# Two MLP channel mixers behind attention: the up projections as seven block products instead of eight, on chunks of 768 tokens

## The chip, the cores and the metric

One core of one Trainium2 chip. The metric is device time of the whole launch in microseconds (us); lower is better. Three runs of the kernel before lie between 791.92 and 793.27 us.

## The reference

Clustered attention on q, k, v of shape (2, 8, 768, 64), then two mixers on the result x (2 batches x 768 tokens x 512 channels), all in fp32:

```python
def _moe_ref(x, U, V, w_ch1, w_ch2):          # w_ch1 512 x 2048
    xt = x.transpose(0, 2, 1)
    u = x + (xt @ U @ V).transpose(0, 2, 1)   # rank 32
    return u + np.maximum(u @ w_ch1, 0.0) @ w_ch2
def _moe2_ref(x, w_tok1, w_tok2, w_ch1, w_ch2):   # w_ch1 512 x 1536
    xt = x.transpose(0, 2, 1)
    h = np.maximum(xt @ w_tok1, 0.0) @ w_tok2     # 768 -> 256 -> 768
    u = x + h.transpose(0, 2, 1)
    return u + np.maximum(u @ w_ch1, 0.0) @ w_ch2
```

The change concerns the products `u @ w_ch1` (the "up" matmuls), and with them everything in the function `mixers`. Attention is the same in both kernels.

## The kernel before

A product of fp32 numbers is made from three passes: each operand is split into a high part (rounded to the matmul's fp32r type, by ScalarE, `ACT`) and a low part (the rest, by VectorE, `DVE`), and TensorE (`PE`) adds high x high, high x low and low x high into one PSUM bank of 512 columns.

The mixers follow each other. Each begins with token mixing (L957, L976: L940 transposes the resulting u into `uT`), and goes on to its channel mixer in three chunks of 512 tokens (`CHUNK`). In a chunk a loop runs over the blocks f of 128 hidden units, 16 of them in the first mixer and 12 in the second. `up(f)` (L989) makes 12 matmuls of 512 columns into one of two banks `hid`; ACT writes relu of it as `h_hi` (L1067), DVE `h_lo` (L1126); `down(f)` (L998) makes 12 matmuls of 512 columns into four accumulators `acc`. The loop is written with the ups one block ahead: up(f+1), down(f), up(f+2), down(f+1). So 84 blocks pass, with 1008 up and 1008 down matmuls. Weights of each block come by two DMAs of 256 KB from SyncE's queue (`SP`, L882 and L884) into double buffers, and are split by ACT (L1039, L1069) and DVE (L1089, L1130). The hidden layer lives for one block only. At the end of a chunk DVE adds the four accumulators to x (L1150). GpSimd (`POOL`) splits V and the token weights (L906 to L919) at the start and tiles of x for the second mixer (L926, L928), far ahead of their use. All order is by hand: each engine has its own list, with semaphores between them.

## Time and profile before

| | |
|---|---|
| median of 3 runs | 792.05 us |
| the profiled execution | 792.6 us |
| its span, first to last instruction | 790.7 us |
| PE busy in the span | 97% |
| DVE, ACT, POOL busy | 57%, 46%, 17% |
| mixers: first PE matmul to the last DVE add | from 269.1 to 788.2 us |

1.9 us of the profiled execution lie around its span. In the profile a matmul's busy time is longer than its turn, since matmuls overlap in the array: what counts is the distance between the starts of one and the next.

### The profile page before, as it was taken

Reading aid. Unit: us, or ns where it says so; the run is one execution under the profiler, and the core shown is the slowest. Engines: PE = TensorE matmul, PEld = TensorE weight load, DVE = VectorE, ACT = ScalarE, POOL = GpSimd, SP = SyncE. Lnnn points to the kernel's source line nnn. Section 1 sums busy time; section 2 is a strip of 40 time slices with the busy share of each in tenths; the row PEclk is TensorE's granted clock in tenths of the full one; section 3 lists DMA queues with packets and bytes.
Section 4 is the critical chain, followed back from the end, with each engine's and each line's share of the span. In section 5 each row is a group of like instructions: output and inputs, shape, how many; then the busy total and the mean of one; then the engine's idle time right before and its main releaser. Section 6 shows DMA issues by size and latency. Waiting matters only on the chain.

```text
span 790.7 us, 12902 instructions
## 1 busy us (share of the span) xinstructions
PE 768.8 (97%) x3997; PEld 659.8 (83%) x3997; DVE 450.1 (57%) x761; ACT 361.7 (46%) x742; POOL 136.0 (17%) x162
## 2 busy tenths in 40 slices
PE   7989999999999889999999999999999999999998
PEld 6878999999999668888888888888888888888886
DVE  4778999999999684333533353334254335334333
ACT  5567888888888533323333233332123233323321
POOL 1351332233228660000300040000300000000000
PEclk9999999999999999999999999999999999999999
DMA  7935354444441223333323323333003333333334
GB/s 246 225 105 134 94 122 103 119 105 119 105 117 33 70 96 101 93 105 83 104 80 106 99 84 110 88 98 106 0 1 107 93 93 94 93 106 84 103 105 173
DMA packets 82840, 81.08 MB, mean 103 GB/s; under 512 B 7296, under 2 KB 69056, under 8 KB 82816
## 3 DMA queue, kind: packets, MB, share of 16 engines
q1 hardware_dynamic: 82816, 80.77, 37.0%
q8 instruction: 14, 0.23, 0.1%
q14 instruction: 10, 0.08, 0.0%
HBM read 56.95 MB, written 4.72 MB: 78 GB/s over the span
## 4 chain that ended last, share of the span: by engine, by line
PE 63%; DVE 2%; ACT 0%; issue 0%
PE bank L998 29%; PE bank L989 29%; PE bank L976 2%; PE bank L957 2%; PE bank L940 1%; DVE kT_hi L1099 1%; DVE x L1117 0%; DVE x L1150 0%; DVE w_lo L1130 0%; DVE uT_lo L1094 0%; DVE w_lo L1089 0%; DVE t L1108 0%; DVE h_lo L1126 0%; ACT qT_hi L1048 0%; ACT h_hi L1067 0%
## 5 line engine op out<-in xcount | busy, mean ns | idle before, releaser
L1126 DVE SCALAR_TENSOR_TENSOR h_lo<-bank,h_hi 128x512 fp32r<-128x512 f32 x84 | 58.1, 692 | 261.8 <-ACT h_hi L1067 261.8
L1067 ACT ACTIVATE h_hi<-bank 128x512 fp32r<-128x512 f32 x84 | 50.2, 598 | 301.4 <-PE bank L989 301.4
L989 PE MATMUL bank<-uT_hi,w_hi 128*128 128x512 f32 x336 | 131.2, 391 | 0.0
L998 PE MATMUL bank<-w_hi,h_hi 128*128 128x512 f32 x336 | 131.1, 390 | 0.0
L989 PE MATMUL bank<-uT_hi,w_lo 128*128 128x512 f32 x336 | 130.8, 389 | 0.0
L989 PE MATMUL bank<-uT_lo,w_hi 128*128 128x512 f32 x336 | 130.8, 389 | 0.0
L998 PE MATMUL bank<-w_hi,h_lo 128*128 128x512 f32 x336 | 130.7, 389 | 0.0
L998 PE MATMUL bank<-w_lo,h_hi 128*128 128x512 f32 x336 | 130.7, 389 | 0.0
L595 DVE TENSOR_TENSOR pT_lo<-back,pT_hi 128x384 fp32r<-128x384 f32 x192 | 98.1, 552 | 6.9 <-ACT pT_hi L496 3.5
L496 ACT ACTIVATE pT_hi<-back 128x384 fp32r<-128x384 f32 x192 | 84.4, 497 | 36.2 <-PE back L740 34.6
L563 DVE TENSOR_REDUCE negmax<-front 128x1 f32<-128x768 f32 x96 | 91.3, 952 | 9.2 <-PE front L639 9.2
L447 ACT ACTIVATE prob<-front,negmax 128x768 f32<-128x768 f32 x96 | 87.9, 916 | 1.2 <-DVE negmax L563 1.2
L740 PE MATMUL back<-ident,prob 128*128 128x128 f32 x576 | 79.3, 274 | 0.4 <-DVE pT_lo L595 0.4
L989 PEld LDWEIGHTS bank<-uT_hi,w_hi 128*128 128x128 f32 x336 | 63.1, 188 | 13.5 <-DVE uT_lo L1094 0.4
L998 PEld LDWEIGHTS bank<-w_hi,h_hi 128*128 128x128 f32 x336 | 63.1, 188 | 13.2 <-issue 0.2
L998 PEld LDWEIGHTS bank<-w_hi,h_lo 128*128 128x128 f32 x336 | 63.1, 188 | 13.1
L989 PEld LDWEIGHTS bank<-uT_hi,w_lo 128*128 128x128 f32 x336 | 63.0, 188 | 13.1
L989 PEld LDWEIGHTS bank<-uT_lo,w_hi 128*128 128x128 f32 x336 | 63.1, 188 | 12.9
L998 PEld LDWEIGHTS bank<-w_lo,h_hi 128*128 128x128 f32 x336 | 63.1, 188 | 12.9
L740 PEld LDWEIGHTS back<-ident,prob 128*128 128x128 f32 x576 | 68.4, 141 | 2.7 <-DVE pT_lo L595 0.6
L758 PE MATMUL back<-pT_hi,v_split 128*128 128x384 f32 x192 | 67.9, 354 | 0.8 <-DVE pT_lo L595 0.6
L760 PE MATMUL back<-pT_lo,v_split 128*128 128x384 f32 x192 | 64.8, 337 | 0.0
(125 smaller groups left out, 1054.1 us busy)
## 6 DMA issues: line engine op xcount, KB each, us to landing
w_raw<-in_moe_w_ch_dram SPq DMA_DIRECT2D x168, 256.0 KB, 2.9
Q<-qT_hi SPq DMA_DIRECT2D x64, 96.0 KB, 2.2
K<-kT_hi SPq DMA_DIRECT2D x64, 96.0 KB, 2.1
q_raw<-in_q_dram SPq DMA_DIRECT2D x8, 384.0 KB, 6.0
k_raw<-in_k_dram SPq DMA_DIRECT2D x8, 384.0 KB, 7.0
Q<-qT_lo SPq DMA_DIRECT2D x32, 96.0 KB, 2.1
K<-kT_lo SPq DMA_DIRECT2D x32, 96.0 KB, 2.1
v_raw<-in_v_dram SPq DMA_DIRECT2D x16, 192.0 KB, 2.7
```

Source lines behind the costliest of these rows:

```text
L447: nc.scalar.activation(prob[t % 2][:, :], s_slot[t % 2], ACT.Exp, bias=negmax[:, t % TPP:t % TPP + 1], accum_out=sums[:, t % TPP:t % TPP + ...
L496: nc.scalar.activation(pT_hi[G % 2][:, HT * half:HT * half + HT, P * (t % GT):P * (t % GT) + P], t_bank[n % 3][:, 0:HT * P].rearrange("p ( ...
L563: nc.vector.tensor_reduce(negmax[:, t % TPP:t % TPP + 1], s_slot[t % 2], AX.X, ALU.max, negate=True).then_inc(max_done, 1)
L595: nc.vector.tensor_tensor(pT_lo[G % 2][own], t_bank[n % 3][:, 0:HT * P].rearrange("p (n c) -> p n c", c=P), pT_hi[G % 2][own].bitcast(F32) ...
L740: last = nc.tensor.transpose(t_bank[i % 3][:, t * P:(t + 1) * P], prob[n % 2][:, c:c + P], ident[:, :])
L758: nc.tensor.matmul(av_bank, v_sp[j][:, token_of(t), :], pT_hi[n % 2][:, t, :], start=(t == 0), stop=False)
L760: last = nc.tensor.matmul(av_bank, v_sp[j][:, token_of(t), :], pT_lo[n % 2][:, t, :], start=False, stop=(t == NT - 1))
L957: last = nc.tensor.matmul(bank_of(L, n)[:, :], w, y[:, i, :], start=(t == 0 and m == 0), stop=(t == NT - 1 and m == len(pairs) - 1))
L989: last = nc.tensor.matmul(hid[par][:, :], w[par][:, kd, :], y[cc % 2][:, kd, :], start=(kd == 0 and m == 0), stop=(kd == KD - 1 and m == 2))
L998: last = nc.tensor.matmul(acc[k][:, :], y[par][:, k * P:(k + 1) * P], w[par][:, :], start=(start and m == 0), stop=(stop and m == 2))
L1067: nc.scalar.activation(h_hi[par][:, :], hid[par][:, :], ACT.Relu).then_inc(h_hi_made, 1)
L1126: nc.vector.scalar_tensor_tensor(out=h_lo[par][:, :], in0=hid[par][:, :], scalar=0.0, in1=h_hi[par][:, :].bitcast(F32), op0=ALU.max, op1=A ...
```

## The change

The chunks become the two batches of each mixer, four chunks `cc` of 768 tokens, and each is done in two phases. In the first, all up products of the chunk: two blocks of 128 hidden units (a pair, `p`; 8 pairs in each chunk of the first mixer, 6 in the second) form, with the two halves of the 512 channels and of the 768 tokens, a product of 2x2 by 2x2 blocks, done by Strassen's scheme in Winograd's form: seven products q of 6 matmuls of 384 columns (42 a pair) with sums on either side. POOL makes the four sums of weight blocks in place (`pair_sums`, L975 to L980), ACT and DVE split all seven in one and two instructions (`a_high`, `a_low`); four sums of blocks of uT and the split of seven (`moving_...`) are made once a chunk, by DVE and ACT for the first, by POOL alone for the three others. A product goes to one of six banks in turn; ACT copies the first (`snap`) and DVE adds the others into `h`, by 7 additions of 384 columns (`combine`). `h` keeps the chunk's whole hidden layer. In the second phase (`down`) each block is split (`hs_hi`, `hs_lo`, 768 columns) and 18 matmuls of 512 columns follow, into six banks. Token mixing and transposes of the next chunk are put between the products of this one (`pieces`: TF the first token matmuls, TS the second, TR the transposes; two banks, 6 and 7, are theirs); for that, POOL splits tiles of x (`stage`) and the second token weights (`second_weights`, two times now). The core of the diff, with indents shortened:

```diff
-            def down(f, par, start=False, stop=False):
-                wait(pe, w2_made, n0 + f + 1)
-                wait(pe, h_made, n0 + f + 1)
-                for k in range(TPC):
-                    for m, (y, w) in enumerate(((h_hi, w2_hi), (h_hi, w2_lo), (h_lo, w2_hi))):
-                        last = nc.tensor.matmul(acc[k][:, :], y[par][:, k * P:(k + 1) * P], w[par][:, :],
-                                                start=(start and m == 0), stop=(stop and m == 2))
-                    if stop:
-                        last.then_inc(acc_mm, 1)
...
-            with pe.Fori(0, nf[L] // 2 - 1) as i:
-                up(i * 2 + 2, 0)
-                down(i * 2 + 1, 1)
-                up(i * 2 + 3, 1)
-                down(i * 2 + 2, 0)
...
-            def rest(f, par):
-                dve.wait_ge(h_hi_made, n0 + f + 1)
-                nc.vector.scalar_tensor_tensor(out=h_lo[par][:, :], in0=hid[par][:, :], scalar=0.0,
-                                               in1=h_hi[par][:, :].bitcast(F32),
-                                               op0=ALU.max, op1=ALU.subtract).then_inc(h_made, 1)
-                dve.wait_ge(w2_hi_made, n0 + f + 1)
-                nc.vector.tensor_tensor(w2_lo[par][:, :], w2_raw[par][:, :],
-                                        w2_hi[par][:, :].bitcast(F32), ALU.subtract).then_inc(w2_made, 1)
...
+def pieces(cc):
+    at = {}
+    if cc == 0:
+        for t in range(NT):
+            at[3 + 2 * t] = [("TR", NT + t)]
+    elif cc < 3:
+        first = 6
+        for t in range(NT):
+            at[first + t] = [("TF", t)]
+            at[first + NT + 2 + t] = ([("TR", NT * (cc + 1) + t - 1)] if t > 0 else []) + [("TS", NT * (cc + 1) + t)]
+        at[first + 2 * NT + 2] = [("TR", NT * (cc + 1) + NT - 1)]
+    return at
...
+    def load_pair(cc, p):
+        n = pbase[cc] + p
+        w3 = layers[cc // B][0].rearrange("(k p) f -> p k f", p=P)
+        wait(sp, a_made, 2 * (n - 1))
+        for i in range(2):
+            f0 = (2 * p + i) * P
+            sp.dma_start(a_raw[n % 2][:, 2 * i:2 * i + 2, :, :].rearrange("p s k c -> p (s k) c"),
+                         w3[:, :, f0:f0 + P]).then_inc(w1_in[n % 2], 16)
...
+        load_w2(cc, 0, 0)
+        load_w2(cc, 1, 1)
+        if cc + 1 < NCH:
+            load_pair(cc + 1, 0)
+            load_pair(cc + 1, 1)
+        with sp.Fori(1, nf[cc] // 2) as i:
+            load_w2(cc, i * 2, 0)
+            load_w2(cc, i * 2 + 1, 1)
...
+    def pair_sums(cc, p):
+        n = pbase[cc] + p
+        raw = a_raw[n % 2]
+        pool.wait_ge(w1_in[n % 2], (n // 2 + 1) * 32)
+        nc.gpsimd.tensor_tensor(raw[:, 4, :, :], raw[:, 2, :, :], raw[:, 3, :, :], ALU.add).then_inc(sums_made, 1)
+        pool.wait_ge(sums_made, 4 * n + 1)
+        nc.gpsimd.tensor_tensor(raw[:, 5, :, :], raw[:, 4, :, :], raw[:, 0, :, :], ALU.subtract).then_inc(sums_made, 1)
+        nc.gpsimd.tensor_tensor(raw[:, 2, :, :], raw[:, 0, :, :], raw[:, 2, :, :], ALU.subtract).then_inc(sums_made, 1)
+        pool.wait_ge(sums_made, 4 * n + 2)
+        nc.gpsimd.tensor_tensor(raw[:, 6, :, :], raw[:, 1, :, :], raw[:, 5, :, :], ALU.subtract).then_inc(sums_made, 1)
...
+    def moving_split(cc, q):
+        if q in BC_SUM:
+            pool.wait_ge(bc_sum, 4 * cc + BC_SUM[q])
+        nc.gpsimd.tensor_copy(bc_hi[:, q, :, :], bc_block[q]).then_inc(bc_hi_made, 1)
+        pool.wait_ge(bc_hi_made, PRODS * cc + q + 1)
+        nc.gpsimd.tensor_tensor(bc_lo[:, q, :, :], bc_block[q], bc_hi[:, q, :, :].bitcast(F32),
+                                ALU.subtract).then_inc(bc_made, 1)
...
+    def moving_blocks(cc):
+        pool.wait_ge(uT_made, NT * (cc + 1))
+        pool.wait_ge(prod_done, PRODS * pbase[cc])
+        moving_sum(cc, tmp2, block_of(0, 1), block_of(0, 0))
+        moving_split(cc, 0)
+        pool.wait_ge(bc_sum, 4 * cc + 1)
...
+    for cc in range(NCH):
+        if cc in (1, 2):
+            for t in range(2):
+                stage(cc + 1, t)
+            second_weights(cc)
+        for p in range(2, npair[cc]):
+            if cc in (1, 2):
+                for t in range(2 * p - 2, min(2 * p, NT)):
+                    stage(cc + 1, t)
+            pair_sums(cc, p)
+        if cc + 1 < NCH:
+            pair_sums(cc + 1, 0)
+            pair_sums(cc + 1, 1)
+            moving_blocks(cc + 1)
...
+    def up(cc, p):
+        n = pbase[cc] + p
+        par = (p + cc) % 2
+        pe.wait_ge(a_made, 2 * (n + 1))
+        for q in range(PRODS):
+            at, out_ = PRODS * p + q, up_bank(p, q)
+            if p == 0:
+                pe.wait_ge(bc_made, PRODS * cc + q + 1)
+            if at >= UPBANKS:
+                product_read(pe, cc, at - UPBANKS)
+            elif cc == 0:
+                pe.wait_ge(u_made, NT + at + 1)
+            else:
+                pe.wait_ge(y_made, NT * (cc - 1) + at + 1)
+            for kt in range(2):
...
+                    last = nc.tensor.matmul(out_[:, 0:GW], w[par][:, A_SLOT[q], kt, :], y[:, q, kt, :],
+                                            start=(kt == 0 and m == 0), stop=(kt == 1 and m == 2))
+            last.then_inc(prod_done, 1)
+            for kind, m in slot_pieces(cc, p, q):
+                piece(cc, kind, m)
...
+    def a_high(cc, p):
+        n = pbase[cc] + p
+        act.wait_ge(sums_made, 4 * (n + 1))
+        if p == 1 and cc > 0:
+            act.wait_ge(acc_mm, NT * cc)
+        else:
+            wait(act, prod_done, PRODS * (n - 1 if p > 0 else n))
+        if (cc, p) == (0, 1):
...
+    def up(cc, p):
+        n = pbase[cc] + p
+        for q in range(PRODS):
+            if q == 0:
+                act.wait_ge(prod_done, PRODS * n + 1)
+                nc.scalar.activation(h_block(p, 1, 1), up_bank(p, q)[:, 0:GW], ACT.Copy).then_inc(snap_done, 1)
+                if p + 1 < npair[cc]:
...
+    def a_low(cc, p, part):
+        n = pbase[cc] + p
+        own = slice(0, 4) if part == 0 else slice(4, PRODS)
+        par = (p + cc) % 2
+        dve.wait_ge(a_hi_made, n + 1)
+        nc.vector.tensor_tensor(a_lo[par][:, own, :, :], a_raw[n % 2][:, own, :, :],
+                                a_hi[par][:, own, :, :].bitcast(F32), ALU.subtract).then_inc(a_made, 1)
...
+    def combine(p, n, q, dst, other):
+        dve.wait_ge(prod_done, PRODS * n + q + 1)
+        nc.vector.tensor_tensor(dst, up_bank(p, q)[:, 0:GW], other, ALU.add).then_inc(comb_done, 1)
+    def up(cc, p):
+        n = pbase[cc] + p
+        c11, c12, c21, c22 = (h_block(p, i, k) for i in range(2) for k in range(2))
+        more = p + 1 < npair[cc]
+        for q in range(PRODS):
+            if q == 1:
+                dve.wait_ge(snap_done, n + 1)
+                combine(p, n, q, c12, c22)
+            elif q == 2:
+                combine(p, n, q, c11, c22)
+            elif q == 3:
+                dve.wait_ge(comb_done, COMBS * n + 1)
+                combine(p, n, q, c21, c12)
+                if more:
+                    a_low(cc, p + 1, 0)
+            elif q == 4:
+                dve.wait_ge(comb_done, COMBS * n + 3)
+                combine(p, n, q, c22, c21)
+                combine(p, n, q, c12, c12)
+            elif q == 5:
+                if more:
+                    a_low(cc, p + 1, 1)
+                dve.wait_ge(comb_done, COMBS * n + 5)
+                combine(p, n, q, c12, c12)
+            elif q == 6:
+                combine(p, n, q, c21, c21)
+            for kind, m in slot_pieces(cc, p, q):
+                piece(cc, kind, m)
+    def down(cc, pair, f, e):
+        F = fbase[cc] + 2 * pair + e
+        dve.wait_ge(w2_hi_made, F + 1)
+        nc.vector.tensor_tensor(w2_lo[cc % 2][e], w2_raw[cc % 2][e], w2_hi[cc % 2][e].bitcast(F32),
+                                ALU.subtract).then_inc(w2_made, 1)
+        dve.wait_ge(hs_hi_made, F + 1)
+        nc.vector.scalar_tensor_tensor(out=hs_lo[:, e, :], in0=h[:, f, :], scalar=0.0,
+                                       in1=hs_hi[:, e, :].bitcast(F32),
+                                       op0=ALU.max, op1=ALU.subtract).then_inc(hs_made, 1)
...
+    for m in range(NT):
+        add_mix(m)
+    for part in range(2):
+        a_low(0, 0, part)
+    dve.wait_ge(uT_made, NT)
+    moving_sum(tmp2, block_of(0, 1), block_of(0, 0))
+    moving_low(0)
+    add_mix(NT)
+    dve.wait_ge(bc_sum, 1)
+    moving_sum(tmp1, block_of(1, 1), tmp2)
+    add_mix(NT + 1)
+    dve.wait_ge(bc_sum, 2)
+    moving_low(1)
+    moving_low(2)
+    add_mix(NT + 2)
+    moving_sum(block_of(0, 1), block_of(1, 1), block_of(0, 1))
+    dve.wait_ge(bc_sum, 3)
+    moving_low(3)
+    moving_low(4)
+    moving_low(5)
+    moving_sum(tmp1, block_of(1, 0), tmp1)
+    dve.wait_ge(bc_sum, 4)
+    moving_low(6)
+    for m in range(NT + 3, 2 * NT):
+        add_mix(m)
...
+            up(cc, p)
+        for e in range(2):
+            down(cc, 0, e, e)
+        if cc + 1 < NCH:
+            for part in range(2):
+                a_low(cc + 1, 0, part)
...
```

On DVE the list of a pair reads so, before, in the loop of a chunk (per turn two blocks of 512 tokens; `w_lo` are low parts of weights, `h_lo` of the hidden block):

```order
L1089 TENSOR_TENSOR w_lo<-w_raw,w_hi 128x512
L1125 REGISTER_ALU
L1126 SCALAR_TENSOR_TENSOR h_lo<-bank,h_hi 128x512
L1130 TENSOR_TENSOR w_lo<-w_raw,w_hi 128x512
L1088 REGISTER_ALU
L1089 TENSOR_TENSOR w_lo<-w_raw,w_hi 128x512
L1126 SCALAR_TENSOR_TENSOR h_lo<-bank,h_hi 128x512
L1130 TENSOR_TENSOR w_lo<-w_raw,w_hi 128x512
```

and now, on DVE, in the last pairs of a chunk's first phase and at the start of its second (`h` from `bank` are the additions, `a_lo` from `a_raw` the low parts of the next pair's weights, `a_lo` from `w_raw` those of a down block's):

```order
L1297 TENSOR_TENSOR h<-bank,h 128x384 x5
L1273 TENSOR_TENSOR a_lo<-a_raw,a_hi 128x1024
L1297 TENSOR_TENSOR h<-bank,h 128x384 x2
L1273 TENSOR_TENSOR a_lo<-a_raw,a_hi 128x768
L1297 TENSOR_TENSOR h<-bank,h 128x384 x9
L1331 TENSOR_TENSOR a_lo<-w_raw,a_hi 128x512
L1334 SCALAR_TENSOR_TENSOR hs_lo<-h,hs_hi 128x768
L1331 TENSOR_TENSOR a_lo<-w_raw,a_hi 128x512
L1334 SCALAR_TENSOR_TENSOR hs_lo<-h,hs_hi 128x768
L1273 TENSOR_TENSOR a_lo<-a_raw,a_hi 128x1024
L1273 TENSOR_TENSOR a_lo<-a_raw,a_hi 128x768
```

The split of the next pair's weights now stands between additions that each wait for a product, and the split of the first down block behind the last addition.

On POOL, which before had nothing between tiles of x here, this list stands now from the end of a down phase's work to the first pairs of the next chunk:

```order
L1002 TENSOR_TENSOR moving_tmp<-uT,moving_tmp 128x768
L1007 CAST bc_hi<-moving_tmp 128x768
L1009 TENSOR_TENSOR bc_lo<-moving_tmp,bc_hi 128x768
L988 CAST qT_lo<-x 128x512
L990 TENSOR_TENSOR qT_lo<-x,qT_lo 128x512
L988 CAST qT_lo<-x 128x512
L990 TENSOR_TENSOR qT_lo<-x,qT_lo 128x512
L996 CAST kT_hi<-wt_raw 128x768
L998 TENSOR_TENSOR kT_hi<-wt_raw,kT_hi 128x768
L996 CAST kT_hi<-wt_raw 128x768
L998 TENSOR_TENSOR kT_hi<-wt_raw,kT_hi 128x768
L988 CAST qT_lo<-x 128x512
```

The splits of uT (before on ACT and DVE), of tiles of x and of the token weights (before early in the mixers) now stand one behind the other on POOL, ahead of the third tile of x.

## Rows read from the trace of the kernel before

**Rows 1.** The page: busy time of each engine, and its share.

```profile
PE 768.8 (97%) x3997; PEld 659.8 (83%) x3997; DVE 450.1 (57%) x761; ACT 361.7 (46%) x742; POOL 136.0 (17%) x162
```

**Rows 2.** The chain that ended last, in order of time: start, us, engine, matmuls.

```profile
425.58 2.72 PE bank L989 x12
...
553.48 16.32 PE bank L957 x72
...
785.47 2.73 DVE x L1150 x4
```

**Rows 3.** Time line around L660, matmuls of 384 columns: start, us.

```profile
35.34 0.34 PE L660 MATMUL front<-kT_lo,c_blk 128*128 128x384 f32 x1
...
37.10 0.34 PE L660 MATMUL front<-qT_hi,c_blk 128*128 128x384 f32 x1
```

**Rows 4.** Groups by line on DVE, ACT, PEld: us, mean ns, idle before.

```profile
L595 DVE TENSOR_TENSOR pT_lo<-back,pT_hi 128x384 fp32r<-128x384 f32 x192 | 98.1, 552 | 6.9 <-ACT pT_hi L496 3.5
L760 PEld LDWEIGHTS back<-pT_lo,v_split 128*128 128x128 f32 x192 | 36.2, 188 | 0.0
L1069 ACT ACTIVATE w_hi<-w_raw 128x512 fp32r<-128x512 f32 x84 | 52.4, 624 | 0.0
L569 DVE SCALAR_TENSOR_TENSOR qT_lo<-back,qT_hi 128x768 fp32r<-128x768 f32 x8 | 7.6, 954 | 5.2 <-ACT qT_hi L465 5.2
```

**Rows 5.** Groups by line on POOL, the same columns.

```profile
L385 POOL TENSOR_TENSOR avsum<-av 128x192 f32<-128x192 f32 x32 | 19.1, 598 | 130.9 <-ACT av L503 130.9
L372 POOL TENSOR_TENSOR v_split<-v_raw,v_split 128x384 fp32r<-128x384 f32 x16 | 16.2, 1015 | 1.3
L926 POOL CAST qT_hi<-x 128x512 fp32r<-128x512 f32 x12 | 8.3, 688 | 242.1 <-DVE x L1150 242.1
L919 POOL TENSOR_TENSOR wt_lo<-wt_raw,wt_hi 128x768 fp32r<-128x768 f32 x2 | 4.5, 2257 | 0.2
L917 POOL CAST wt_hi<-wt_raw 128x768 fp32r<-128x768 f32 x2 | 3.3, 1640 | 0.0
```

**Rows 6.** Time line of the start of the mixers, DVE and POOL.

```profile
269.76 6.57 DVE L1099 TENSOR_TENSOR kT_hi<-x,qT_hi 128x512 fp32r<-128x512 f32 x6 [3.37 <-ACT qT_hi L1048]
270.82 2.55 POOL L908 TENSOR_TENSOR qT_lo<-V_raw,qT_lo 128x768 fp32r<-128x768 f32 x1
279.09 3.68 DVE L1117 TENSOR_TENSOR x<-bank,x 128x512 f32<-128x512 f32 x6 [0.23 <-PE bank L976]
280.50 1.47 POOL L911 CAST qT_lo<-wt_raw 128x1536 fp32r<-128x1536 f32 x1 [7.13 <-DMA wt_raw<-in_moe_w_tok_dram]
291.11 2.24 POOL L919 TENSOR_TENSOR wt_lo<-wt_raw,wt_hi 128x768 fp32r<-128x768 f32 x1
291.52 2.38 DVE L1130 TENSOR_TENSOR w_lo<-w_raw,w_hi 128x512 fp32r<-128x512 f32 x1
```

**Rows 7.** DMA issues: KB each, median us to landing.

```profile
w_raw<-in_moe_w_ch_dram SPq DMA_DIRECT2D x168, 256.0 KB, 2.9
wt_raw<-in_moe_w_tok_dram SPq DMA_DIRECT2D x2, 768.0 KB, 8.1
```

**Rows 8.** Time line of the first matmuls of the mixers.

```profile
269.12 0.47 PE L957 MATMUL bank<-qT_hi,qT_lo 128*128 128x512 f32 x1 [2.20 <-PEq L95]
...
271.14 0.63 PE L957 MATMUL bank<-kT_hi,qT_lo 128*128 128x512 f32 x1
271.57 0.63 PE L957 MATMUL bank<-qT_hi,qT_lo 128*128 128x512 f32 x1
...
287.19 0.50 PE L989 MATMUL bank<-uT_hi,w_hi 128*128 128x512 f32 x1
```

**Rows 9.** Stretches: PE, PEld, DVE, ACT, POOL busy, PEclk, DMA share, GB/s.

```profile
271.00:272.00 1.00, 1.00 (x4) 0.71 (x4) 1.00 (x2) 1.00 (x3) 1.00 (x1) 0.50 0.96 316
272.00:273.00 1.00, 1.00 (x4) 0.80 (x3) 1.00 (x1) 0.33 (x1) 1.00 (x1) 0.50 0.18 53
...
300.00:400.00 100.00, 100.00 (x450) 82.95 (x450) 39.82 (x62) 31.67 (x58) 7.90 (x8) 1.00 0.34 98
```

More of the change, by code:

```diff
@@ L801, in mixers @@
[L801 to L805 removed]
+        h = sb("h", [P, 2 * NPAIR, S])
+        moving_tmp = sb("moving_tmp", [P, NPAIR, S])
+        bc_hi = sb("bc_hi", [P, PRODS, 2, GW], F32R)
+        bc_lo = sb("bc_lo", [P, PRODS, 2, GW], F32R)
@@ new lines, in token_first @@
+            def token_first(cc, t):
+                n = (cc - 2) * NT + t
+                if t == 0:
+                    pe.wait_ge(uT_made, NT * cc)
+                    pe.wait_ge(wt1_made, 2)
+                pe.wait_ge(st_made, n + 1)
+                for r in range(NR):
+                    cols = slice(r * P, (r + 1) * P)
+                    for m, (w, y) in enumerate(((wt1_hi, st_hi), (wt1_hi, st_lo), (wt1_lo, st_hi))):
+                        last = nc.tensor.matmul(bank[6 + r][:, :], w[:, t, cols], y[t % 2], start=(t == 0 and m == 0),
+                                                stop=(t == NT - 1 and m == 2))
+                last.then_inc(tile_mm, 1)
@@ new lines, in token_second @@
+            def token_second(m):
+                cc, t = m // NT, m % NT
+                cols = slice(t * P, (t + 1) * P)
+                pe.wait_ge(tok_made, B + NR * (cc - 1))
+                if t == 0:
+                    pe.wait_ge(wt2_made, 2 * NR * (cc - 1))
+                else:
+                    pe.wait_ge(u_made, m)
+                for r in range(NR):
+                    for n, (w, y) in enumerate(((wt2_hi, t2_hi), (wt2_hi, t2_lo), (wt2_lo, t2_hi))):
+                        last = nc.tensor.matmul(bank[6][:, :], w[:, r, cols], y[:, r, :], start=(r == 0 and n == 0),
+                                                stop=(r == NR - 1 and n == 2))
+                last.then_inc(mix_mm, 1)
@@ new lines, in down @@
+            def down(cc, f, e, start=False, stop=False):
+                F = fbase[cc] + f
+                pe.wait_ge(w2_made, F + 1)
+                pe.wait_ge(hs_made, F + 1)
+                done = PRODS * npair[cc]
+                for k in range(NT):
+                    if start:
+                        k = (done + k) % UPBANKS
+                        product_read(pe, cc, max(at for at in range(done) if at % UPBANKS == k))
+                    cols = slice(k * P, (k + 1) * P)
+                    for m, (y, w) in enumerate(((hs_hi, w2_hi), (hs_hi, w2_lo), (hs_lo, w2_hi))):
+                        last = nc.tensor.matmul(bank[k][:, :], y[:, e, cols], w[cc % 2][e],
+                                                start=(start and m == 0), stop=(stop and m == 2))
+                    if stop:
+                        last.then_inc(acc_mm, 1)
+                if not stop:
+                    last.then_inc(down_mm, 1)
```

525 lines of the change are left out of this document (276 added, 249 removed).

## The prediction

> **What bounds the kernel now.** I read the page first: PE is busy nearly the whole span, DVE just over half, POOL a sixth [rows 1]. Then the chain that ended last: through the mixers it is PE's and nothing else, 12 matmuls in 2.72 us, so 0.2267 us from one to the next, through channel mixers and token mixing alike [rows 2]. From 300 to 400 us PE is busy for all of 100 us, DVE for 40 [rows 9]. So time is PE's count of columns, and whatever makes PE wait is added in full. The reader should look for two things: how many columns go, and what each of the new waits costs on engines that today wait for PE.
>
> **What goes.** For 768 tokens and a pair of hidden blocks there are now 36 up matmuls: 36 x 0.2267 = 8.16 us. The change makes 42 of 384 columns. From 35.34 to 37.10 us ten such matmuls start in attention, 0.176 us each [rows 3]: 7.39 us a pair. Over 28 pairs 28 x 0.77 = **21.6 us less**. Down, token matmuls and transposes keep their number and width. The gain is 0.77 us a pair and not an eighth of 8.16 (1.02), because a narrower matmul spreads its fixed part over fewer columns. By the Trainium skill, TensorE: Matmul & The Clock Gate, "Wait — 56ns, not 53.3ns?", starts lie N / 2.4 GHz + 2.5 ns apart at full clock, 0.2157 us for 512 columns; this trace shows 0.2267, so I go by the rows. By that rule the gain would be 28 x (7.77 - 6.83) = 26 us.
>
> **New wait 1, at the start of each pair.** PE begins pair p+1 only when DVE has made both parts of its low weights, and in DVE's list they stand behind additions that wait for products. DVE's prices: 384 wide 0.55 us, 768 wide 0.95 [rows 4], so 1.05 ns a column and 1.22 us for 1024; in a row each takes 0.08 less (six additions of 512 in 3.68 us, 0.61 each [rows 6], where one alone would be 0.69). Counted from a pair's first matmul: the fourth product's last matmul starts at 23 x 0.176 = 4.05, takes 0.34 [rows 3], and with 0.03 for the semaphore (my estimate from the starts of such readers) DVE goes on at 4.42. Then addition 0.47, first part 1.14, two additions 0.94, second part 0.95: 7.92, and PE restarts at about 8.0, 0.6 us after it has run out of work at 7.39.
>
> This is without POOL. POOL makes the weight sums of pair p+2, four additions of 256 columns: between 0.60 for 192 and 1.02 for 384 columns [rows 5], 2.17 ns a column, 0.74 each, about 2.9 together. Their DMAs are issued when pair p starts, land some 3.3 us later (2.9 [rows 7] and the first one's issue), and so POOL adds from about 3.4 to 6.3, while DVE wants to begin the first part at 4.9. The two get in each other's way: of DVE's six splits L1099, which take 0.6 each alone, the series took 6.57 us while POOL ran L906 and L908, and L1130 took 2.38 us instead of 0.69, ending 0.55 after POOL's L919; but DVE's additions from a PSUM bank went at 0.61 beside POOL's L911 [rows 6]. So a DVE instruction with both inputs in SBUF waits for the end of POOL's running one, and one that reads a bank does not. For `a_low` that is up to 0.74 us, 0.45 on average when it happens. I take it for half of the 24 pair starts within chunks (not where POOL is late or has no more pairs), so 0.6 + 0.2: 24 x 0.8 = **19 us**. The six banks are no limit: each was filled six products earlier. ACT's split of 1792 columns (0.62 for 512 [rows 4], by 0.83 ns a column 1.7 us) is ready at 3.4, before DVE wants it.
>
> **New wait 2, from up to down, four times.** Before, down(f) had its inputs a block ahead. Now, behind the last product, come its end 0.19, addition 0.55, `w2_lo` 0.6, `hs_lo` 0.95: 2.3 us of idle PE. In three of the four, POOL is then at the sums of the next chunk's pairs and goes on with `moving_blocks`, 7 casts of about 0.85 and 11 two-input instructions of about 1.85 (768 columns, by rows 5's slope), and all four DVE splits of a pair of down blocks have both inputs in SBUF. The first wait becomes about 2.9. Then DVE's list has the 1024 and 768 wide splits of the next chunk's first pair, whose ACT part must wait for those sums, between the second down block and the third: with POOL between each two, DVE reaches block 2 some 2.4 us after PE wants it. For nine more blocks a DVE pair needs 1.55 us and up to two POOL instructions (2.7) of the 4.08 us PE takes; together another 1.8 us. 3 x 7.1 + 2.3 = **23.5 us**. No row has an instruction of `hs_lo`'s form with both inputs in SBUF. If it does not wait for POOL, each of the three falls to about 4 us and the term to 14; I take that it waits, since the nearest rows, splits with the same two inputs [rows 6], do. By the Trainium skill, GPSIMD Engine Reference, "Specifications", contention is with DVE instructions in a 2-port mode "or with two SBUF inputs"; by that rule the term is 23.5 and not 14. The trace agrees for the splits it has.
>
> **New wait 3, POOL ahead of token mixing, chunks 1 and 2.** The second token weights are loaded when the last down phase ends: 8.1 us to land [rows 7], then 2 x (1.64 + 2.26) [rows 5] = 7.8, then a tile of x, cast 0.69 and split 1.29 by that slope, 1.9 in a row, with DVE's collisions 18.4 us into the chunk. PE wants this third tile after 9 products and 2 token tiles, 9 x 1.056 + 2 x 1.36, with its other waits 14: it waits 4.4. The fifth comes behind the sums of pair 2 and another tile: 1.7, the sixth 0.5. 2 x 6.6 = **13 us**. Before, PE passed this stage without a gap (L957) [rows 2].
>
> **New wait 4, the first chunk's start.** PE's first up matmul came 18.1 us after the mixers' first matmul [rows 8]. Now four sums and seven splits of 768 columns (11 x 0.87) stand in DVE's list between the additions that free the banks: product 3 needs the addition for tile 9, behind all of them. Starting at 11.3, DVE has 6 + 3 + 1 additions (6.1), `a_low` twice (2.0, and 2.5 behind POOL's split of 1536 columns, 3.5 us by 2.17 ns a column), 9.6 for sums and splits, and some 3.5 of waits for POOL, ACT and transposes: product 3 starts at 35.0 and not at 21.3. That is 13.8 us; behind its first up the old start lost, by my estimate, 1.8 us: **+12**.
>
> **The clock.** After 2.2 us of idle PE before 269.12 [rows 8] the granted clock was 0.50 from 271 to 273 [rows 9], the 1.2 GHz level, and matmuls of 512 started 0.43 apart instead of 0.227 [rows 8]. With the parts of the microseconds on either side I estimate 3.4 us at this level; half of it is lost, 1.7 us. The new kernel has about twelve waits of 2.2 us or more (one or two at each up-to-down step, two in wait 3, three at the start). Each may cost 1.7 us; I take four, **7 us**, since a slow stretch within the up phase partly fills time that PE would wait for DVE.
>
> **Sum.** -21.6 + 19 + 23.5 + 13 + 12 + 7 = +53. Attention and the tail (additions of 0.69 us, then stores) stay as they are. The span becomes 790.7 + 53 = 843.7, 1.9 lie around it, and the median of before is 0.5 under its profiled execution: **845 us**, 6.7% slower.
>
> **Rivals.** (a) POOL and DVE do not hold each other up as rows 6 suggest, or only rarely: pair starts cost 24 x 0.6 = 14, up to down 4 x 2.3 = 9, wait 3 12, the start 10, the clock 3: with -21.6 that is +26, 818 us. For it: rows 6 have only a few such meetings. Against it: all of them agree. (b) Other side, faster: PE's list stays the bound and only the four ends of up phases show, -21.6 + 9 = -12.4, 780 us. It decides from the point where all new waits together fall under 21.6 us of the 74.5 I count; the place is `a_low` before pair starts, which would have to be finished by 7.39 and POOL's third tile by 14 us. For it: DVE's busy sum in the up phase (7 x 0.47 + 2.1 = 5.4 us a pair) is less than 7.39, so a list in better order would fit. Against it: the order is fixed, and with DVE's column time halved, up to down (4 x 1.4), a start of 5 and wait 3 of 12 remain, +1, 793 us. (c) The clock falls at every long gap, twelve times (8 x 1.7 = 14 more), and every pair start meets POOL (24 x 0.2 = 5 more): +72, 864 us. (d) The change does not do what it says: matmuls of 384 columns are held by the weight load, 0.188 us [rows 4], not 0.176. Then no more than 28 x (8.16 - 7.90) = 7 us go, while the pair's chain lengthens by 24 x 0.012 = 0.3 and leaves 0.6 at a pair start, 14 in all: -7 + 14 + 23.5 + 13 + 12 + 7 = +63, 855 us. Against it: rows 3 and 4 are of the same weights and width, at 0.176.
>
> **How the numbers follow.** Forecast 0.62, (a) 0.17, (b) 0.07, (c) 0.07, (d) 0.05, no difference within 0.2% 0.02. The range goes from 808, which is (a) with half of its cost at the start and in wait 3 hidden, to 862, just under (c). The forecast's own range is 832 to 858. 0.2% (1.6 us) is about what a measurement of this kernel can tell from no change: faster 0.07, same 0.02, slower 0.91.
>
> **What the new profile would show.** Up matmuls at 0.176 and 8.4 to 8.5 us from pair to pair, PE waiting for DVE `a_lo`; DVE instructions at `a_lo` and `hs_lo` far longer than 0.95 to 1.22 us at their worst, those into `h` at 0.55 always; 3 us of idle PE before down and again before its third block; 4 us waits for POOL in chunks 1 and 2; product 3 of the first chunk about 35 us into the mixers; stretches of clock 0.50. What would make me wrong: pairs at 7.4 us, or `a_lo` never longer than its columns cost.

## The result, and the profile after

The changed kernel takes 842.13 us (median of 4 runs, 840.15 to 847.78) against 792.6 us. The estimated ratio is 1.0635, 95% interval 1.0611 to 1.0659 (the two medians give 1.0625). It is 49.5 us slower; 845 was forecast. Its profiled execution, from which the rows come, was the longest of the four (span 846.0 us; the others 838.2 to 841.4, with a mean granted clock of 0.978 to 0.984 where this one had 0.965). Of its 55.3 us over the span of before 2.4 lie in attention, where the stretch at the 0.50 level is longer (mean clock 0.66 from 50 to 60 us, before 0.83), and 2.3 in the stores at the end.

From the page of after, the engines, PE's group of the up matmuls, DVE's of the additions and of the second operand of down, and the chain by engine:

```profile
PE 772.3 (91%) x4165; PEld 689.5 (81%) x4165; DVE 596.5 (71%) x860; ACT 364.8 (43%) x665; POOL 348.5 (41%) x332
PE 42%; DVE 17%; issue 3%; POOL 3%; DMA 1%; ACT 1%; DVEq 0%; POOLq 0%; ACTq 0%
L1297 DVE TENSOR_TENSOR h<-bank,h 128x384 f32<-128x384 f32 x196 | 104.1, 552 | 98.3 <-PE bank L1144 98.2
L1144 PE MATMUL bank<-bc_hi,a_hi 128*128 128x384 f32 x392 | 137.4, 350 | 24.5 <-DVE a_lo L1273 13.8
L1334 DVE SCALAR_TENSOR_TENSOR hs_lo<-h,hs_hi 128x768 fp32r<-128x768 f32 x56 | 82.8, 1479 | 4.2 <-ACT hs_hi L1235 3.2
```

PE's busy share went from 97 to 91% [rows 1] and the chain, which was almost PE's alone through the mixers [rows 2] (DVE 2% of the span), now goes through DVE for a sixth of the span. The additions (L1297) read a bank and take 0.55 us always; `hs_lo` (L1334), with both inputs in SBUF, has a mean of 1.48 where 768 columns cost 0.95 [rows 4].

The same in stretches (start, up and down of the four chunks), columns as in [rows 9]:

```profile
271.00:293.00 22.00, 17.20 (x72) 13.14 (x72) 19.99 (x19) 10.46 (x16) 16.10 (x13) 0.81 0.31 94
293.00:375.80 82.80, 68.59 (x360) 65.17 (x360) 58.46 (x88) 27.49 (x32) 28.66 (x31) 0.89 0.19 56
375.80:447.00 71.20, 68.14 (x289) 55.12 (x290) 48.44 (x37) 19.16 (x28) 38.76 (x23) 0.98 0.17 51
447.00:540.00 93.00, 82.22 (x434) 76.23 (x433) 53.36 (x83) 24.19 (x28) 43.59 (x44) 0.96 0.21 61
540.00:611.00 71.00, 68.02 (x289) 54.90 (x289) 48.24 (x37) 19.15 (x28) 38.50 (x23) 0.98 0.17 51
611.00:686.00 75.00, 66.75 (x349) 61.36 (x347) 40.58 (x64) 19.79 (x24) 34.44 (x35) 0.95 0.21 60
686.00:739.70 53.70, 51.53 (x217) 41.65 (x218) 39.78 (x30) 13.91 (x21) 41.31 (x25) 0.97 0.24 71
739.70:791.20 51.50, 45.20 (x254) 43.31 (x252) 35.35 (x57) 13.52 (x15) 11.77 (x12) 1.00 0.19 59
791.20:846.00 54.80, 49.23 (x216) 40.43 (x216) 21.96 (x28) 13.68 (x20) 0.00 (x0) 0.98 0.24 77
```

PE's idle time lies in the up phases and at their ends. The granted clock is below 1.00 in all stretches but one: length times (1 - clock) times 2, summed, is 53 us at the 0.50 level, where the old kernel's mixers had about 3.4.

The pitch of the up matmuls, from the second to the last of a pair (40 starts further on):

```profile
357.22 0.34 PE L1144 MATMUL bank<-bc_lo,a_hi 128*128 128x384 f32 x1
...
364.15 0.34 PE L1144 MATMUL bank<-bc_hi,a_lo 128*128 128x384 f32 x1
```

That is 0.1733 us from start to start, and not the 0.176 of the rows of attention.

The time line of after in three places, DVE and POOL side by side. A pair start (PE's last matmul of the pair started at 519.67, and it went on at 520.92):

```profile
517.47 1.28 DVE L1273 TENSOR_TENSOR a_lo<-a_raw,a_hi 128x1024 fp32r<-128x1024 f32 x1
518.68 1.01 DVE L1297 TENSOR_TENSOR h<-bank,h 128x384 f32<-128x384 f32 x2
519.61 1.25 DVE L1273 TENSOR_TENSOR a_lo<-a_raw,a_hi 128x768 fp32r<-128x768 f32 x1
517.63 1.72 POOL L978 TENSOR_TENSOR a_raw<-a_raw 128x256 f32<-128x256 f32 x1
519.31 0.73 POOL L980 TENSOR_TENSOR a_raw<-a_raw 128x256 f32<-128x256 f32 x1
520.92 0.45 PE L1144 MATMUL bank<-bc_hi,a_hi 128*128 128x384 f32 x1 [0.91 <-DVE a_lo L1273]
```

The last split of the weights is what PE waits for, and it takes 1.25 us instead of 0.95: it ends 0.8 us after POOL's L980. POOL's L978 in turn takes 1.72 instead of 0.73: it ends 0.6 us after DVE's first split, which was over at 518.75. From up to down, first chunk:

```profile
374.27 1.48 DVE L1334 SCALAR_TENSOR_TENSOR hs_lo<-h,hs_hi 128x768 fp32r<-128x768 f32 x1
378.21 4.33 DVE L1273 TENSOR_TENSOR a_lo<-a_raw,a_hi 128x1024 fp32r<-128x1024 f32 x2
382.51 2.30 DVE L1331 TENSOR_TENSOR a_lo<-w_raw,a_hi 128x512 fp32r<-128x512 f32 x1
384.73 2.58 DVE L1334 SCALAR_TENSOR_TENSOR hs_lo<-h,hs_hi 128x768 fp32r<-128x768 f32 x1
377.44 2.53 POOL L1002 TENSOR_TENSOR moving_tmp<-uT 128x768 f32<-128x768 f32 x1
379.92 1.82 POOL L1007 CAST bc_hi<-uT 128x768 fp32r<-128x768 f32 x1
381.82 2.44 POOL L1009 TENSOR_TENSOR bc_lo<-uT,bc_hi 128x768 fp32r<-128x768 f32 x1
375.85 0.47 PE L1161 MATMUL bank<-a_hi,hs_hi 128*128 128x512 f32 x1 [3.26 <-issue]
387.46 0.47 PE L1161 MATMUL bank<-a_hi,hs_hi 128*128 128x512 f32 x1 [1.57 <-DVE hs_lo L1334]
```

DVE's two splits for the next chunk and the 0.68 us one behind them take 6.6 us instead of 2.7 while POOL makes the moving blocks, and block 2 comes late. The third tile of x in chunk 1:

```profile
452.08 2.43 POOL L996 CAST kT_hi<-wt_raw 128x768 fp32r<-128x768 f32 x1 [3.74 <-DMA wt_raw<-in_moe_w_tok_dram]
...
461.25 0.61 POOL L988 CAST qT_lo<-x 128x512 fp32r<-128x512 f32 x1
461.94 1.26 POOL L990 TENSOR_TENSOR qT_lo<-x,qT_lo 128x512 fp32r<-128x512 f32 x1
```

POOL waits 3.74 us for the second token weights, then splits them for 9.2 us; the tile is ready at 463.20 and PE, idle for 4.0 us, goes on at 463.25.

**The balance of the mixers.** They took 519.1 us from their first matmul to the end of the last DVE addition (269.12 to 788.2) and now take 569.6 (271.57 to 841.16): +50.5. At 0.1733 us a start, a pair without a wait takes 7.28 us, and so it does in kernels 1, 8 and 9 below, start to start; 28 x (8.16 - 7.28) = 24.6 us less. The distances between PE's matmuls beyond 0.176 and 0.2267 us each, group by group: pair starts 16.7, which is 18.7 against 7.28, since the first matmul behind each of the 18 waits is followed by the next after 0.28 us and not 0.173; up to down 6.9 + 6.8 + 5.2 + 2.3 = 21.2; the third tile 2 x 4.2 = 8.4; the first chunk's start 4.6 + 1.0 + 6.0 = 11.5, less 1.8 of the old one, 9.7. With -24.6 that is +33.4. The rest is 17.1 us. Nearly all of it is matmuls at 1.2 GHz: in the stretches at the 0.50 level their starts, outside the waits, lie 17.2 us further apart than at full clock, before 1.5.

### The profile page after: what moved, and what is told of

Read it like the earlier page. It is cut to its first block, busy times and chain, and to the rows that moved or that the text cites. A ratio compares the mean times of both kernels' runs of the same rounds, so it can differ in the third digit from the quotient of the medians.

```text
span 846.0 us, 13004 instructions
## 1 busy us (share of the span) xinstructions
PE 772.3 (91%) x4165; PEld 689.5 (81%) x4165; DVE 596.5 (71%) x860; ACT 364.8 (43%) x665; POOL 348.5 (41%) x332
## 4 chain that ended last, share of the span: by engine, by line
PE 42%; DVE 17%; issue 3%; POOL 3%; DMA 1%; ACT 1%; DVEq 0%; POOLq 0%; ACTq 0%
PE bank L1161 21%; PE bank L1144 17%; DVE a_lo L1273 5%; DVE hs_lo L1334 3%; DVE h L1297 3%; PE bank L1101 2%; PE bank L1087 2%; DVE a_lo L1331 2%; POOL kT_hi L998 1%; DMA wt_raw<-in_moe_w_tok_dram 1%; PE bank L1116 1%; POOL kT_hi L996 1%; DVE kT_hi L1348 1%; DVE bc_lo L1343 1%; DVE x L1280 1%
## 5 line engine op out<-in xcount | busy, mean ns | idle before, releaser
L1297 DVE TENSOR_TENSOR h<-bank,h 128x384 f32<-128x384 f32 x196 | 104.1, 552 | 98.3 <-PE bank L1144 98.2
L1144 PE MATMUL bank<-bc_hi,a_hi 128*128 128x384 f32 x392 | 137.4, 350 | 24.5 <-DVE a_lo L1273 13.8
L1161 PE MATMUL bank<-a_hi,hs_hi 128*128 128x512 f32 x336 | 134.0, 399 | 19.2 <-issue 9.4
L1144 PE MATMUL bank<-bc_hi,a_lo 128*128 128x384 f32 x392 | 134.1, 342 | 0.0
L1144 PE MATMUL bank<-bc_lo,a_hi 128*128 128x384 f32 x392 | 134.0, 342 | 0.0
L1161 PE MATMUL bank<-a_hi,hs_lo 128*128 128x512 f32 x336 | 133.0, 396 | 0.0
L1161 PE MATMUL bank<-a_lo,hs_hi 128*128 128x512 f32 x336 | 132.5, 394 | 0.0
L1144 PEld LDWEIGHTS bank<-bc_hi,a_hi 128*128 128x128 f32 x392 | 75.6, 193 | 33.3 <-DVE a_lo L1273 19.6
L975 POOL TENSOR_TENSOR a_raw<-a_raw 128x256 f32<-128x256 f32 x28 | 23.9, 853 | 171.6 <-DMA a_raw<-in_moe_w_ch_dram 171.6
L1334 DVE SCALAR_TENSOR_TENSOR hs_lo<-h,hs_hi 128x768 fp32r<-128x768 f32 x56 | 82.8, 1479 | 4.2 <-ACT hs_hi L1235 3.2
L1144 PEld LDWEIGHTS bank<-bc_lo,a_hi 128*128 128x128 f32 x392 | 75.8, 193 | 1.2
L1273 DVE TENSOR_TENSOR a_lo<-a_raw,a_hi 128x1024 fp32r<-128x1024 f32 (+1 forms) x56 | 75.3, 1351 | 0.0
```

The source lines that it names most:

```text
L1144: last = nc.tensor.matmul(out_[:, 0:GW], w[par][:, A_SLOT[q], kt, :], y[:, q, kt, :], start=(kt == 0 and m == 0), stop=(kt == 1 and m == 2))
L1161: last = nc.tensor.matmul(bank[k][:, :], y[:, e, cols], w[cc % 2][e], start=(start and m == 0), stop=(stop and m == 2))
L1273: nc.vector.tensor_tensor(a_lo[par][:, own, :, :], a_raw[n % 2][:, own, :, :], a_hi[par][:, own, :, :].bitcast(F32), ALU.subtract).then_in ...
L1297: nc.vector.tensor_tensor(dst, up_bank(p, q)[:, 0:GW], other, ALU.add).then_inc(comb_done, 1)
L1334: nc.vector.scalar_tensor_tensor(out=hs_lo[:, e, :], in0=h[:, f, :], scalar=0.0, in1=hs_hi[:, e, :].bitcast(F32), op0=ALU.max, op1=ALU.sub ...
```

## The experiments

The theory (A): the narrower matmuls gain what was forecast, and the loss is a set of separate waits that come from the order of DVE's and POOL's lists and from their mutual hold-ups, plus slow clock behind them. The rivals: (B) the clock is the main loss and can be removed by itself; (C) POOL or DVE is short of time, so that a wait removed in one place comes back in another; (D) collisions matter little. Each ratio is against runs of the kernel before that were taken beside it.

**1. The low weights of the next pair ahead of the additions.** In DVE's list, `a_low` part 0 right behind the second addition of the pair, part 1 behind the third:

```diff
@@ up(cc, p) on DVE, q == 2 and 3
                         combine(p, n, q, c11, c22)
+                        if more:
+                            a_low(cc, p + 1, 0)
...
                         if more:
-                            a_low(cc, p + 1, 0)
+                            a_low(cc, p + 1, 1)
...
                     elif q == 5:
-                        if more:
-                            a_low(cc, p + 1, 1)
```

> The split of the next pair's weights moved ahead in VectorE's list: its first part behind the addition of product 2 instead of 3, its second behind the addition of product 3 instead of in front of product 5's. Theory A (TensorE waits at pair starts for VectorE's list): chain 3.36 + 0.47 + 1.14 + 0.47 + 0.87 = 6.3 us, ahead of the pair's end at 7.39, so the 18 waits on a_lo, 16.6 us together, go and the time is about 826 us. Rival B (what is lost is the granted clock, the waits only come with it): stretches at half clock stay where they are, at most 3 us less. Rival C (collisions with GpSimd decide at pair starts): the moved splits collide as before, a third of the 16.6 us stays, about 831 us.

Measured: 822.97 us, ratio 1.038 (1.0356 to 1.0404), 19 us less than the changed kernel. Time line of this kernel's DVE between two pairs:

```profile
512.83 1.22 DVE L1273 TENSOR_TENSOR a_lo<-a_raw,a_hi 128x1024 fp32r<-128x1024 f32 x1
513.96 0.55 DVE L1297 TENSOR_TENSOR h<-bank,h 128x384 f32<-128x384 f32 x1
514.43 0.95 DVE L1273 TENSOR_TENSOR a_lo<-a_raw,a_hi 128x768 fp32r<-128x768 f32 x1
515.29 2.07 DVE L1297 TENSOR_TENSOR h<-bank,h 128x384 f32<-128x384 f32 x4
```

No wait of PE's for `a_lo` at L1273 is left. DVE does the same work; only its place in the list was wrong. Not all of the gain is pair starts: the steps from up to down also fell, from 21.2 to 17.7 us. The clock hardly changed (mean granted clock of the mixers 0.96 in both traces), so the waits could be taken away with the slow stretches left in place, which speaks against (B).

**2. POOL no longer makes the moving blocks.** ACT makes the high parts and DVE the sums and low parts, one piece behind a down block:

```diff
@@ GpSimd, end of a chunk's up phase
-                    moving_blocks(cc + 1)
@@ ACT and DVE, behind down block f
+MOVES = {2: [("s", 0)], 3: [("l", 0), ("s", 1)], 4: [("l", 1)], 5: [("l", 2), ("s", 2)], 6: [("l", 3)],
+         7: [("l", 4)], 8: [("l", 5)], 9: [("s", 3)], 10: [("l", 6)]}
```

> The four sums and seven splits of the moving blocks of chunks 1 to 3 are taken from GpSimd and given to ScalarE (casts) and VectorE (0.95 us each, one behind a down block). Theory A (GpSimd holds up VectorE's two-input SBUF splits): although VectorE gets 10 us more to do in each of three down phases, TensorE's waits behind an up phase fall from about 6.9, 6.8 and 5.2 us to about 3.6 each; with 3 us less at half clock, 842 becomes 832 us. Rival D (no collision, VectorE's own time decides): 3 x 10 us more on VectorE leaves the waits or lengthens them, 842 to 850 us.

Measured: 835.31 us, ratio 1.0548 (1.0519 to 1.0578). DVE got 33 pieces more, of about 0.95 us, and its other groups got cheaper:

```profile
L1318 DVE SCALAR_TENSOR_TENSOR hs_lo<-h,hs_hi 128x768 fp32r<-128x768 f32 x56 | 57.3, 1024 | 2.1
L1378 DVE TENSOR_TENSOR bc_lo<-uT,bc_hi 128x768 fp32r<-128x768 f32 x12 | 11.4, 951 | 0.0
```

`hs_lo` is back from 1479 to 1024 ns, 25.5 us in all, and behind the first wait of about 3 us no wait is left in a down phase. That speaks for collisions and against (D). The forecast was 832. The steps from up to down fell by 9.7 us, to 3.2, 3.0, 3.0 and 2.3, but some 2.5 came back in waits for `a_lo` at pair starts, one of them new.

**3. PE kept busy from up to down.** Twenty transposes of `ident` into bank 7 ahead of `down(cc, 0, 0)`.

> 20 transposes of the identity into an unused bank (20 x 0.109 = 2.2 us) are put on TensorE between the last up product and the first down matmul, where it waits 3.2 us anyway. Rival B (the clock is a cost of its own): the stretches of 3.4 us at half clock behind these places go, 3 x 1.7 = 5 us less, 837 us, and if long waits elsewhere cost the same, 16 us of the loss are clock. Theory A alone (waits, clock beside the point): no difference, 842 us within 1.

Measured: 842.81 us, ratio 1.0631 (1.0613 to 1.0649), no change. The slow stretch behind the first wait was gone in all three chunks, and in two of them another stood at the next wait, where DVE was late anyway. Here the clock gave nothing by itself.

**4. The weight sums left out** (from the third pair on POOL makes none, so the products use the wrong weights and the output is not the reference's):

```diff
@@ pair_sums(cc, p) on GpSimd
+                if n >= 2:
+                    return
```

> GpSimd's sums of weight blocks are left out from the third pair on (ScalarE splits what lies there, so the values are not the reference's). Theory A: a wait at a pair start is 0.52 to 0.6 us of VectorE's order and up to 0.6 of collision with these sums; without them every pair start shows 0.5 to 0.6, 24 of them 13 us instead of 16.6, the first wait behind an up phase falls by about 0.5, and GpSimd reaches its tiles of x 3 us earlier in chunks 1 and 2 for the fifth tile only: 836 to 838 us. If collisions are nothing: 842.

Measured: 846.69 us, ratio 1.0679 (1.0661 to 1.0698): 4.6 us slower with less work, a miss. POOL and DVE at the first end of an up phase:

```profile
370.23 1.81 POOL L1004 TENSOR_TENSOR moving_tmp<-uT 128x768 f32<-128x768 f32 x1 [81.89 <-PE bank L1146]
371.98 1.29 POOL L1009 CAST bc_hi<-uT 128x768 fp32r<-128x768 f32 x1
370.59 2.00 DVE L1334 TENSOR_TENSOR a_lo<-w_raw,a_hi 128x512 fp32r<-128x512 f32 x1
374.01 2.32 DVE L1334 TENSOR_TENSOR a_lo<-w_raw,a_hi 128x512 fp32r<-128x512 f32 x1
```

The pair starts did shrink, to 0.69 us each in 15 of 18 cases. But POOL, with no sums left, began the moving blocks at once, and DVE's splits for the first down blocks met instructions of 1.3 to 2.4 us and not of 0.73: the waits from up to down rose to 7.9, 7.9 and 8.0 us. That is 4.8 us more, and the pair starts are 3.4 less, so these two explain only 1.4 of the 4.6; where the rest comes from is not shown.

**5 to 7. Three waits, one at a time.** The fifth has the second token weights loaded and split in the down phase before. The sixth has, at the start, the additions of tiles 6 to 11 ahead of all sums and splits of the moving blocks, and POOL splits the first token weights later, behind pair 3's sums. The seventh has DVE's splits for the first down block ahead of two additions, and those for the next chunk's first pair, ACT's too, at the end of the down phase. Of each, part of the edit:

```diff
@@ 5: GpSimd
-                    second_weights(cc)
...
                     moving_blocks(cc + 1)
+                    if cc < 2:
+                        second_weights(cc + 1)
@@ 6: DVE, start
+            for m in range(NT, 2 * NT):
+                add_mix(m)
             dve.wait_ge(uT_made, NT)
@@ 7: DVE, up(cc, p), q == 4
+                        if not more:
+                            down(cc, 0, 0, 0)
```

> The second token weights are loaded in the middle of the previous down phase into rows of the hidden array that are used late, and their splits are made by POOL behind its making of the moving blocks, in the down phase, no longer ahead of the tiles of x of chunks 1 and 2. If the 4.2 us before the third tile of x in chunks 1 and 2 come from POOL having the weight splits ahead of that tile, both gaps go (8.4 us), while POOL stays busy some 8 us longer in two down phases, in which DVE's splits meet it: I give back about 1.5 us each in the chunks 0 and 1. Sum -5.5 us: 836 to 838. If the tiles are late for another reason (their own load, the cast on DVE's side), the gaps stay and the time is 842 to 845.

> Only the first chunk's start: in DVE's list all six additions that make tiles 6 to 11 of the mixed x stand ahead of the sums and splits of the moving blocks, and POOL splits the first token weights later, so it does not hold DVE there. If product 3 waits at 34.9 us for DVE's list as such, the order moves the 4.6 and 6.0 us gaps about but the list has the same length, less the collisions with POOL: product 3 comes 1 to 5 us earlier, 837 to 841. If the slow start is held by the clock of the 20.5 us stretch and not by DVE, nothing changes in the time (842 to 843), since the stretch stays as it is.

> At the end of each up phase DVE makes the first down block's two low parts ahead of the additions of products 5 and 6 where they do not need them, and the splits for the next chunk's first pair move from the start of the down phase to its end. If the four steps from up to down cost what DVE has in its list ahead of the first blocks, the sums of 6.9, 6.8, 5.2 and 2.3 us fall to about 4.5, 4.5, 4 and 0.7: 833 to 835. If they are set by POOL alone (its moving blocks run whatever DVE's order is), the first gap stays near 3.3 us and what is gained behind the second block is lost later: 839 to 843.

Measured: 837.45 (1.0541, 1.0519 to 1.0563), 841.65 (1.0598, 1.057 to 1.0625) and 833.44 us (1.0495, 1.0476 to 1.0514). The fifth took both waits of 4.2 us away, left 1.2 + 0.4 in the place of each and added 1.5 to each of two down phases, as expected. The sixth is nearly level with the changed kernel, its interval meets the other's. In its trace the waits of the start are 4.8 + 1.5 + 2.9 instead of 4.6 + 1.0 + 6.0 us, and the fourth pair begins 2.0 us earlier, at 58.1 instead of 60.0 us after the mixers' first matmul: the order of the same list moved the waits more than it shortened them. The seventh made the up-to-down steps 3.9, 3.9, 5.1 and 0.8 us.

**8. All of them** (1, 2, 5, 6, 7 together).

> All edits together: the low weights made before the additions at pair starts, moving blocks made by ACT and DVE in the down phase, the down blocks' splits first, the start and the token weights as in the three others. If the loss is the sum of these independent waits, they take away 16.6 (pair starts), about 17 of 21.2 (up to down), 8.4 (third tiles) and 1 to 4 at the start, and half of the 16 us of slow clock behind those waits: 790 to 798, level with before's 792. If the waits are not independent (what one edit frees is lost at the next wait, or the clock falls as often as before), it stays above 805. If the narrower matmuls did not gain the 21.6 us, it can't come under 812.

Measured: 795.67 us, ratio 1.004 (1.0024 to 1.0056). 46.5 us come back, more than the 19.2 + 6.8 + 4.7 + 0.5 + 8.7 = 39.9 of the five edits one by one. So in sum no wait came back in another place, which refutes (C), though single ones had (experiments 2 and 5).

**9, 10. The waits that were left.** In kernel 8's trace PE still lost 4.8 + 1.5 + 2.5 us at the start, 1.3, 1.6, 1.4 and 0.8 before down, 1.2 + 1.0 for tiles in two chunks, and 1.5 in two down phases. The ninth rearranges the start once more (three additions ahead of the sums and splits, the others between them; ACT splits the second pair's weights earlier, POOL's sums wait for the moving blocks). It makes the first down block's low parts one product earlier and POOL's sums of pair 2 ahead of the third tile, and gives the splits of the second token weights to ACT and DVE. The tenth has all of that but the start, which stays as in kernel 8. Part of the edits, against kernel 8:

```diff
@@ DVE: start (9 only); up(cc, p), q == 3
-            for m in range(NT, 2 * NT):
+            for m in range(NT, NT + 3):
                 add_mix(m)
...
                         if more:
                             a_low(cc, p + 1, 1)
+                        else:
+                            down(cc, 0, 0, 0)
@@ GpSimd, a chunk's pairs
+                    if p == 2:
+                        pair_sums(cc, p)
                     if cc in (1, 2):
```

> On top of the kernel with all edits together. (1) At the start, product 0's low block comes behind three additions and one sum instead of six additions, the others alternate with the additions that free the banks, ACT splits the second pair's weights early, and POOL's sums wait until the blocks are made: by the prices of the profile product 3 starts near 296 instead of 303.4, product 7 about 5 us earlier, and less of it lies in slow clock: -5 to -8 us. (2) The first down block's low parts are made behind product 3 of the last pair, not 4: the four gaps of 1.3, 1.6, 1.4 and 0.8 us before the down phases go, -4.5. (3) POOL makes the sums of pair 2 ahead of the third tile of x, while it has nothing else: the gaps of 1.24 and 0.99 in chunks 1 and 2 go, -4.4. (4) The second token weights are split by ACT and DVE: the gap of 1.48 before a down block goes twice, -3. Sum -17 to -20 against 795.7 if the waits add up one by one: 776 to 779, 2% faster than before. If the losses were only passed on (POOL's or DVE's time is the limit, not its order), it stays at 790 or above.

> As e9_best, but with the first chunk's start left as in the kernel with all edits together: parts (2), (3) and (4) alone, -12 from 795.7, so 783 to 785 and 5 to 8 us above e9_best. If the start is held by the clock and not by DVE's order, e9_best and e10_rest come out the same.

Measured: 778.01 (0.9812, 0.9788 to 0.9836) and 782.52 us (0.9856, 0.9833 to 0.9879). Number 9 is 1.9% faster than the kernel before, and its whole interval lies below 1. PE's longest waits in its mixers, by what they waited for (us, times, longest):

```profile
PE bank L1093 <- DVE x L1271: 2.8, 1, 2.8
PE bank L1040 <- DVE kT_hi L1341: 2.6, 4, 1.4
PE bank L1121 <- issue: 2.3, 1, 2.3
PE bank L1121 <- DVE bc_lo L1336: 1.4, 1, 1.4
```

**11. PE kept busy at the start.** In the changed kernel, 34 transposes before product 0 and 46 before product 3.

> The changed kernel with PE kept busy in the two long waits of the first chunk's start: 34 transposes of the identity matrix into an unused bank before product 0 and 46 before product 3, at 0.11 us each at full clock. DVE's list is as it was, so product 3 can't come before 34.9 us after the mixers' start. If the 20.5 us of half clock there come from PE's idle time ahead of them, that stretch goes or shrinks, and what PE does behind product 3 up to 311.5 us (5.6 busy us of 7) takes about half: 3 us less, 838 to 840. If the clock falls whatever PE does there, the transposes take 0.22 us each, 17.6 us in 10.6 us of waits, and the time is 845 to 850. If the half clock behind product 3 costs nothing because DVE is late again at the next pair start anyway, the stretch goes and the time stays 842 to 843.

Measured: 840.95 us, ratio 1.0603 (1.058 to 1.0627). The same place in windows, first after, then this kernel:

```profile
299.00:305.00 6.00, 1.67 (x6) 1.16 (x4) 4.04 (x6) 3.60 (x6) 0.72 (x1) 0.50 0.00 0
305.00:312.00 7.00, 5.64 (x20) 5.58 (x21) 5.52 (x10) 2.11 (x2) 0.00 (x0) 0.53 0.00 0
```

```profile
299.00:305.00 6.00, 4.35 (x38) 4.14 (x37) 5.02 (x8) 3.37 (x4) 0.00 (x0) 1.00 0.00 0
305.00:312.00 7.00, 6.87 (x44) 6.45 (x43) 5.76 (x10) 1.95 (x4) 0.00 (x0) 1.00 0.14 40
```

The clock stayed at 1.00, and the last matmul of the third pair came 1.9 us earlier, counted from the mixers' first matmul. In the time it is 1.2 us, less than the two intervals can tell apart. All nine other traces of kernels with this start or one close to it (after, 1 to 8) have a slow stretch here, and this one has none. So PE's idle time does bring the clock down here, but of the slow stretch only some 2 us were on the path; the rest lies beside DVE's work.

## Why the prediction was right, step by step

- **The gain, 21.6 us**: the right term, 3 us too small: 24.6. The ten matmuls of attention that gave 0.176 were not quite as dense as the up phases, at 0.1733; the prediction's other figure, 26, lay nearer. Kernel 9 gives a second look: its mixers from the first matmul to the end of the span take 504.3 us (270.5 to 774.8) against 521.6 (269.1 to 790.7), 17.3 less. Its waits at the start are 7.0 against the old 1.8, those in token mixing 3.3 against 1.4, and -24.6 + 5.2 + 1.9 = -17.5. Rival (d), the weight load as the limit, is out: PEld's mean is 193 ns and the pitch is 0.1733 all the same.
- **Wait 1, pair starts, 19 us**: 18.7 (16.7 beyond a pitch of 0.176). Of the 19 that came back in experiment 1, some 3.5 lay in the steps from up to down. The list without collisions gives 0.68 us, not 0.6; 18 of the 24 starts waited (the first of a chunk lie beside slow matmuls or token mixing), 11 of them longer than 0.68 by 0.3 to 0.6; 12 were taken.
- **Wait 2, up to down, 23.5 us**: 21.2. The forecast 2.9, 2.4 and 1.8 for the three parts were 3.4, 1.7 and 1.8 in the first chunk, and 2.3 for the last chunk was 2.3. The open question, whether `hs_lo` waits for POOL, is settled: 2.60 us at worst. By the Trainium skill, GPSIMD Engine Reference, "Specifications", a DVE instruction with two SBUF inputs contends with GpSimd; this trace agrees (0.95 alone, 2.60 beside POOL).
- **Wait 3, 13 us**: 8.4. The third tile was 4.2 us late (4.4 forecast); the 1.7 and 0.5 for the fifth and sixth did not appear. Both times the clock was at 0.50 for 6.8 us from the third tile's wait on (mean 0.57 from 461 to 469 us), and the slower PE gave POOL time to catch up. In experiment 6, chunk 1, the clock was at 1.00 there, and PE waited 2.1, 1.7 and 0.4 us for tiles. So the time saved here is counted again in the clock; no run separates the two.
- **Wait 4, the start, 12 us**: 9.7 of waits, and product 3 at 34.8 us where 35.0 was said.
- **The clock, 7 us**: the term that was most mis-sized, about 16 (15.7 in the matmul starts, 17.1 as the rest of the balance). The step that failed is "I take four": the clock was at 0.50 at or behind seven of the eight new gaps of 2 us or more (not four of twelve), at both third tiles for twice the 3.4 us, and at the start from 291 to 311 us. Rival (c)'s price for the clock, 7 + 14, was nearer; its other half, a collision at every pair start, did not come. I priced a stretch by the single one of the old kernel, which had a single wait ahead of it; here PE's short bursts between the two long waits of the start did not bring the clock back.
- Three errors cancelled, and that the sum fits so well is in part luck: 10 us too little for the clock (17.1, not 7), 9.5 too much for the waits (58.0, not 67.5), 3 too little for the gain. Also, the sum fits the mixers of the longest execution, +50.5; attention and the stores, put at nothing, brought 4.7 more there. Rival (a), no collisions, is refuted by experiment 2, rival (b) by experiment 1; but (b)'s remark that a list in better order would fit was borne out by kernel 9.

What stays open is how the 16 us divide: experiments 3 and 11 show that part of the slow clock costs nothing because DVE is late anyway, and no run removed all of it and left the waits. The 16 us are those of the longest execution; the three others had a higher mean clock and took 4.6 to 7.8 us less, so the clock probably cost less in them.
